# Scores of a gated linear attention: from three matmuls a chunk over zero-padded queries to eight, on two halves of TensorE's rows

## What is computed

```
for t in range(S):
    m_new = maximum(f_gate[t] + m, i_gate[t])
    f_stab = exp(f_gate[t] + m - m_new); i_stab = exp(i_gate[t] - m_new); m = m_new
    C = f_stab * C + i_stab * outer(v[t], k[t])
    n = f_stab * n + i_stab * k[t]
    y[t] = sigmoid(o_gate[t]) * (C @ q[t]) / max(|n . q[t]|, 1)
x = y as [B, S, H * D]
h = relu(x.T @ w_tok1) @ w_tok2;  u = x + h.T
out = u + relu(u @ w_ch1) @ w_ch2
```

## Time and profile before

| | us |
|---|---|
| median of three runs | 455.25 (454.03 to 457.1) |
| the profiled execution's own time | 455.49 |
| its span in the trace | 453.8 |
| TensorE (PE) busy | 439.6, 97% of the span |
| VectorE (DVE) busy | 255.6, 56% |
| ScalarE (ACT) busy | 209.1, 46% |
| GpSimd (POOL) busy | 208.3, 46% |
| granted TensorE clock | 0.995 of full |

### The profile page before, as it was taken

One profiled execution on the slowest core, in us unless ns is written; L12 is line 12 of the kernel. 1 busy time (PEld: TensorE's weight loads), 2 busy tenths in 40 slices (PEclk: granted clock), 3 DMA queues, 4 the chain that ended last, 5 costly groups with the idle time before them and its releaser, 6 DMA issues.

```text
span 453.8 us, 9518 instructions
## 1 busy us (share of the span) xinstructions
PE 439.6 (97%) x3463; PEld 407.6 (90%) x3463; DVE 255.6 (56%) x592; ACT 209.1 (46%) x517; POOL 208.3 (46%) x293
## 2 busy tenths in 40 slices
PE   8899999999999999899999999999999999999996
PEld 3588988999999989799999998899999998999996
DVE  7689865777765356776674237666665326213122
ACT  3666459666554247654552137655652213211120
POOL 7535421789886333888861204798883000000000
PEclk9899999999999999999999999999999999999999
DMA  7557990443344415434454013534310010000101
GB/s 211 195 168 217 348 263 27 119 129 111 103 131 146 127 43 166 143 92 131 124 154 143 1 44 102 150 120 142 126 61 1 1 43 2 0 1 0 46 1 43
DMA packets 36616, 47.38 MB, mean 104 GB/s; under 512 B 3356, under 2 KB 29082, under 8 KB 36570
## 3 DMA queue, kind: packets, MB, share of 16 engines
q1 hardware_dynamic: 35674, 45.76, 33.4%
q10 hardware_dynamic: 896, 1.02, 0.6%
HBM read 42.73 MB, written 4.03 MB: 103 GB/s over the span
## 4 chain that ended last, share of the span: by engine, by line
PE 85%; DVE 5%; issue 4%; ACT 4%; DMA 1%; DVEq 0%; POOL 0%; POOLq 0%; ACTq 0%
PE pC L1165 32%; PE pA L1236 7%; PE pA L1237 7%; PE pA L1238 7%; PE pS L1077 6%; PE pA L1165 5%; PE pY L1134 4%; PE pA L1240 3%; PE pA L1241 3%; PE pC L1015 2%; PE pY L1113 2%; PE pN L1089 2%; DVE gb L856 1%; PE pA L1195 1%; DMA x<-o_gate_dram 1%
## 5 line engine op out<-in xcount | busy, mean ns | idle before, releaser
L988 DVE SCALAR_TENSOR_TENSOR h_lo<-pA,h_hi 128x384 fp32r<-128x384 f32 x96 | 53.5, 557 | 147.9 <-ACT h_hi L760 147.9
L760 ACT ACTIVATE h_hi<-pA 128x384 fp32r<-128x384 f32 x96 | 46.8, 488 | 138.7 <-PE pA L1241 138.6
L1165 PE MATMUL pC<-wc_hi,h_hi 128*128 128x320 f32 x288 | 94.1, 327 | 1.1 <-DVE wc_lo L846 1.0
L1165 PE MATMUL pC<-wc_lo,h_hi 128*128 128x320 f32 x288 | 88.7, 308 | 0.0
L1165 PE MATMUL pC<-wc_hi,h_lo 128*128 128x320 f32 x288 | 88.4, 307 | 0.0
L494 POOL TENSOR_TENSOR gb<-gb,pb 128x384 f32<-128x384 f32 (+1 forms) x54 | 49.1, 909 | 63.9 <-ACT pb L628 63.4
L1236 PE MATMUL pA<-uT_hi,wc_hi 128*128 128x384 f32 x192 | 65.2, 340 | 0.3 <-DVE wc_lo L846 0.3
L1237 PE MATMUL pA<-uT_lo,wc_hi 128*128 128x384 f32 x192 | 64.7, 337 | 0.0
L1238 PE MATMUL pA<-uT_hi,wc_lo 128*128 128x384 f32 x192 | 64.3, 335 | 0.0
L1165 PEld LDWEIGHTS pC<-wc_hi,h_hi 128*128 128x128 f32 x288 | 54.0, 188 | 2.3 <-DVE h_lo L988 1.3
L1165 PEld LDWEIGHTS pC<-wc_lo,h_hi 128*128 128x128 f32 x288 | 54.2, 188 | 0.1
(11 more groups left out here) (135 smaller groups left out, 881.6 us busy)
## 6 DMA issues: line engine op xcount, KB each, us to landing
gb<-g_dram SPq DMA_DIRECT2D x18, 512.0 KB, 3.9
kv<-kvN_dram SPq DMA_DIRECT2D x24, 324.0 KB, 4.0
kd<-kT_dram SPq DMA_DIRECT2D x24, 180.0 KB
qz<-qT_dram SPq DMA_DIRECT2D x72, 60.0 KB
out_dram<-u SPq DMA_DIRECT2D x24, 160.0 KB, 1.9
qd<-qT_dram SPq DMA_DIRECT2D x20, 180.0 KB, 2.6
gq<-g_dram SPq DMA_DIRECT2D x45, 60.0 KB
wc_raw<-w_ch_dram SPq DMA_DIRECT2D x6, 384.0 KB, 6.1
```

Source lines behind the costliest of these rows:

```text
L760: nc.scalar.activation(h2[0][:, slot % 2], pA[slot % 2][:, 0:HALF], ACT.Relu).then_inc(h2_hi, 1)
L988: nc.vector.scalar_tensor_tensor(h2[1][:, slot % 2], pA[slot % 2][:, 0:HALF], 0.0, h2[0][:, slot % 2].bitcast(F32), ALU.max, ALU.subtract) ...
L1165: ins = mm(dst, a[p], b[q], start=first and n == 0, stop=last and n == 2)
```

## The change

Queries and keys now lie in one tensor `kq` with the even heads on rows 0 to 39 and the odd heads on rows 64 to 103, 128 columns for each pair of heads, keys and queries side by side. The host lays the input out that way (`kq_pairs`), and two DMAs of a chunk, 4 KB for each of 40 rows, replace the four. The memset of `qz` is gone, and SP no longer waits for it; SP loads `kq` of chunk 0 first, then the values of chunk 0, and then waits until the output gates of batch 0 have landed before it goes on with chunk 1.

All eight heads' scores of a chunk are made in the step g0 by eight matmuls of 128 columns, even and odd heads by turns. Even heads go to `pS`, odd ones to another bank: `pC[0]` in the first batch, `pN` in the others. They wait until VectorE has read all scores of the chunk before (`p_ready`), and in batches 1 to 3 also until it has read that chunk's last state.

Since `pN` holds the odd heads' scores, the states of batches 1 to 3 are written into columns of `pN` whose scores were read: group 0's in the step g1, those of groups 1 and 2 both in the step g2. VectorE reads the scores of a step in two instructions, one per bank; in g1 it first waits for the state matmul of group 0, in g2 for all three.

```diff
-        kd = sb("kd", [ROWS, R, NG, L])
-        qz = sb("qz", [ROWS, R, NG, GH, L])
+        kq = sb("kq", [128, R, 2, H // 2, L])
...
+        def scores_place(ba, head):
+            pair, odd = divmod(head, 2)
+            return (pC[0] if ba == 0 else pN) if odd else pS, pair * L
+
+        def state_place(ba, g):
+            col = L if ba > 0 and g == NG - 1 else 0
+            return pN[0:HEADS[g] * D, col:col + HEADS[g] * E1]
...
+        def states_in(ba, m):
+            if ba == 0:
+                return [m - 1] if 1 <= m <= STEPS - NG else []
+            c, g = divmod(m, NG)
+            if c >= NC - 1 or g == 0:
+                return []
+            return [m - 1] if g == 1 else [m - 1, m]
...
-                    sp.wait_ge(s_mm, NG * (n - R + 1))
+                    sp.wait_ge(s_mm, n - R + 1)
...
-                sp.dma_start(kd[:, r], kT[ba, c]).then_inc(ready, 16)
-                for j in range(GH):
-                    rows_j = slice(j * D, (j + 1) * D)
-                    sp.dma_start(qz[rows_j, r, :, j, :], queries[rows_j, :, :]).then_inc(ready, 16)
+                for odd in range(2):
+                    sp.dma_start(kq[64 * odd:64 * odd + D, r], kq_pairs[ba, c, odd]).then_inc(ready, 16)
...
+            load_scores(0, 0)
             load_values(0, 0)
-            sp.wait_ge(mem_ready, 1)
-            load_scores(0, 0)
+            for half in range(2):
+                sp.wait_ge(o_in[half], 16)
...
-            nc.vector.memset(qz[:, :, :, :, :], 0.0).then_inc(mem_ready, 1)
...
-                dve.wait_ge(s_mm, k + 1)
+                dve.wait_ge(s_mm, NC * ba + c + 1)
+                if ba > 0 and c < NC - 1 and g > 0:
+                    dve.wait_ge(n_mm, NG * (NC - 1) * ba + NG * c + (1 if g == 1 else NG))
                 dve.wait_ge(e_exp, k + 1)
...
+                for odd in range(2):
+                    heads = [h for h in range(GH * g, GH * g + n) if h % 2 == odd]
+                    tile = gb[:, c % Q, heads[0]:heads[-1] + 1:2, :]
+                    where, col = scores_place(ba, heads[0])
+                    sums = where[:, col:col + len(heads) * L].rearrange("p (h t) -> p h t", t=L)
+                    last = nc.vector.tensor_tensor(tile, sums, tile, ALU.mult)
+                last.then_inc(p_ready, 1)
...
+            def chunk_scores(ba, c):
+                n = NC * ba + c
+                r = c % R
+                pe.wait_ge(qk_in[r], 16 * QK_DMAS * (ba * (NC // R) + c // R + 1))
+                if n > 0:
+                    pe.wait_ge(p_ready, NG * n)
+                if ba > 0:
+                    pe.wait_ge(n_read, states(ba, c - 1))
+                for head in range(H):
+                    pair, odd = divmod(head, 2)
+                    rows = slice(64 * odd, 64 * odd + D)
+                    last = mm(scores_of(ba, head), kq[rows, r, 0, pair, :], kq[rows, r, 1, pair, :],
+                              start=True, stop=True)
+                last.then_inc(s_mm, 1)
...
-                if ks != 0:
+                if ba == 0 and ks != 0:
                     pe.wait_ge(n_read, ks)
+                if ba > 0:
+                    pe.wait_ge(p_ready, STEPS * ba + NG * c + (1 if g == 0 else 2))
+                    if g > 0:
+                        pe.wait_ge(n_read, NG * (NC - 1) * ba + NG * c + 1)
...
-                if m < STEPS:
-                    step_scores(ba, m)
+                if m < STEPS and m % NG == 0:
+                    chunk_scores(ba, m // NG)
```

More of the change, by code:

```diff
@@ L79, in step_in, with program @@
     return slot - BEHIND if b == 0 else slot + AHEAD
-def program(nc, qT, kT, kvN, i_gate, f_gate, o_gate, w_tok1, w_tok2, w_ch1, w_ch2, out):
+def program(nc, kq_pairs, qT, kvN, i_gate, f_gate, o_gate, w_tok1, w_tok2, w_ch1, w_ch2, out):
     ctx = ExitStack()
@@ L163, in program, with scores_of @@
         pN = bank("pN")
-        def scores_bank(ba, m):
-            return [pS, pC[0]][m % 2] if ba == 0 else pS
+        def scores_place(ba, head):
[4 more added lines that the diff above has]
+            return pN[0:HEADS[g] * D, col:col + HEADS[g] * E1]
+        def scores_of(ba, head):
+            where, col = scores_place(ba, head)
+            return where[:, col:col + L]
         def turned_bank(s):
@@ L188, in program @@
         out_done = [sem(f"out_done{i}") for i in range(2)]
-        mem_ready = sem("mem_ready")
         ident_ready = sem("ident_ready")
@@ L303, in program @@
         O_PARTS = ((0, NC - 2), (NC - 2, NC))
-        QK_DMAS = 4
+        QK_DMAS = 2
         GQ_DMAS = 3
@@ L317, in load_scores @@
                 if n >= R:
-                    sp.wait_ge(s_mm, NG * (n - R + 1))
+                    sp.wait_ge(s_mm, n - R + 1)
                 ready = qk_in[r]
-                queries = qT[ba, c]
-                sp.dma_start(kd[:, r], kT[ba, c]).then_inc(ready, 16)
-                for j in range(GH):
-                    rows_j = slice(j * D, (j + 1) * D)
-                    sp.dma_start(qz[rows_j, r, :, j, :], queries[rows_j, :, :]).then_inc(ready, 16)
+                for odd in range(2):
+                    sp.dma_start(kq[64 * odd:64 * odd + D, r], kq_pairs[ba, c, odd]).then_inc(ready, 16)
             def load_decays(ba, c):
@@ L874, in state @@
                 new, old = st[0:n * D, (c + 1) % 2, g, 0:n, :], st[0:n * D, c % 2, g, 0:n, :]
-                sums = pN[0:n * D, 0:n * E1].rearrange("p (h e) -> p h e", e=E1)
+                sums = state_place(ba, g).rearrange("p (h e) -> p h e", e=E1)
                 keep = blocks[0:n * D, 0:n, :]
@@ L928, in attention @@
                     scores(ba, m)
-                if 1 <= m <= STEPS - NG:
-                    state(ba, m - 1)
+                for done in states_in(ba, m):
+                    state(ba, done)
                 c = chunk_at(ba, m, 0) if (ba, m) != (0, NG - 1 + FIRST_LAG) else None
@@ L1086, in step_state @@
                 pe.wait_ge(v_weighed, (NC - 1) * ba + c + 1)
-                if ks != 0:
+                if ba == 0 and ks != 0:
                     pe.wait_ge(n_read, ks)
-                mm(pN[0:n * D, 0:n * E1], kv[:, r, GH * g * D:(GH * g + n) * D],
+                if ba > 0:
+                    pe.wait_ge(p_ready, STEPS * ba + NG * c + (1 if g == 0 else 2))
+                    if g > 0:
+                        pe.wait_ge(n_read, NG * (NC - 1) * ba + NG * c + 1)
+                mm(state_place(ba, g), kv[:, r, GH * g * D:(GH * g + n) * D],
                    vw[:, c % 2, GH * g:GH * g + n, :].rearrange("p h e -> p (h e)"),
@@ L1152, in attention @@
                                 spread_query_decays(k // NG + 1)
-                if 1 <= m <= STEPS - NG:
-                    step_state(ba, m - 1)
+                for done in states_in(ba, m):
+                    step_state(ba, done)
                 if lag(ba) <= m < STEPS + lag(ba):
@@ L1279, in rows, with paired @@
         return np.ascontiguousarray(padded.reshape(B, NG, ROWS, NC, L).transpose(0, 3, 2, 1, 4))
+    def paired(a):
+        return a.reshape(B, H // 2, 2, NC, L, D).transpose(0, 3, 2, 5, 1, 4)
     def by_partition(w, k):
@@ L1289 @@
     arrays = {
-        "qT": rows(q), "kT": rows(k),
+        "kq_pairs": np.ascontiguousarray(np.stack([paired(k), paired(q)], axis=4)),
+        "qT": rows(q),
         "kvN": np.ascontiguousarray(np.concatenate([tokens(k).reshape(B, S, DM), values.reshape(B, S, H * E1)], axis=2)),
```

3 lines of the change are left out of this document (removed).

## The result

The changed kernel takes 466.7 us (median of 4 runs, 465.11 to 467.19) against 454.92 us (4 runs, 454.03 to 457.1): a ratio of 1.0246, 95% interval 1.0202 to 1.029. It is slower. The forecast was 450.6 us with a range from 446.5 to 460.5; the result is outside it. The profiled execution took 467.19 us. Here and in the experiments the ratio and its interval compare with the kernel before and leave out executions more than 1.5% above the fastest of the same kernel, while medians and ranges take in all.

The account below looks back on a forecast made before the run. It took TensorE's instruction stream, except its few waits, to bound the kernel. Terms +0.1 - 3.2 - 2.0 + 0.7 - 0.6 + 0.3 = -4.7 us, from about 455.25, gave 450.6 us, range 446.5 to 460.5.

Parts of the forecast that it names:

- 1.31 us a chunk, made of 0.98 + 0.09 + 0.09 + 0.15: Scores' cost: nine time steps 0.98, entering 0.09, leaving 0.09, bare weight loads 0.15; gain 0.40 us a chunk.
- The first rival: Halves do not run side by side, loads or streaming one after another: 1.93 to 2.1 us a chunk, 458 to 462; chance 0.25.
- the last (no cost at all): Rival: mode changes cost nothing and loads stay hidden, 1.0 us a chunk, 447 us; chance 0.13.
- Chunks 2 to 5 of batches 2 and 3: Full gain of the scores in these chunks: 8 x 0.40 = -3.2 us.
- Batch 1 was to gain 1.3 us: Batch 1: five chunks gain 0.40 us each, -2.0; chunk 2, where VectorE is late, costs +0.7.
- 0.6 us to spare: At g0, VectorE's last state read was to be over by 215.3, PE to arrive at 215.9: no wait.
- the second rival: Halves run side by side, but PE waits in g2 or at g0: 454 to 457 us; chance 0.17.
- chunks 0 and 1 of batches 2 and 3: No gain, as these stretches end in PE's wait at 188.47; VectorE's extra instructions add +0.1 us.
- the slack: In g2, PE's margin behind `p_low` shrinks from 1.3 to 0.3 us; occasional waits counted as 0.3 us in all.
- The wait near 188 us: Batch 2's PE wait, which faster scores only lengthen: a sign to check, 2 us or more.
- the term "-0.6" for batch 0: Batch 0: shorter chain to the scan and earlier gates, less VectorE's 4 x 0.15 us: -0.6 us.
- The prediction's last sentence: Prediction is wrong if batch 0 loses over 1 us, since PE needs a chunk's three reads before the next.

Follow-up runs that it names:

- experiment 2: Kernel before the change, but batch 0's scores use one bank instead of two by turns: 457.88 us, ratio 1.0074.
- experiment 3: Changed kernel, but batch 0's score matmuls contract all 128 rows, same order and banks, scores come out wrong: 455.77 us, ratio 1.0025.
- experiment 6: Changed kernel with VectorE's two products of the values in batch 0 done for one head of eight: 453.67 us, ratio 0.9944.
- e5_apart: Changed kernel with all even heads' score matmuls first, then all odd ones, in all batches: 478.07 us, ratio 1.0523.
- e12_gates: Changed kernel with SP waiting for batch 0's output gates before it issues any scores or values: 470.44 us, ratio 1.0334.
- experiment 4: Changed kernel plus full-height bf16 dummy matmuls in batch 0: ten once 464.11 us, five ahead of chunks 1 to 5 458.91, two ahead of decay spreadings 458.84.
- the hybrid: Batch 0 as in the kernel before, batches 1 to 3 as in the changed kernel: 450.6 us, ratio 0.9912 against the kernel before.
- experiment 7: All even heads' score matmuls first, then all odd ones: 458.84 us in the hybrid, 478.07 us in the changed kernel.
- e14_once: Changed kernel with one block of ten full-height 512-column dummy matmuls ahead of chunk 4's scores in batch 0: 464.11 us, ratio 1.0188.
- e13_full: The run of experiment 3, the changed kernel with batch 0's scores on all 128 rows: 455.77 us, ratio 1.0025.

## Why the prediction was right and wrong

**The scores, right.** Predicted were 1.31 us a chunk, made of 0.98 + 0.09 + 0.09 + 0.15. Measured are 0.10 to enter, 1.09 for the instructions and 0.06 that the next one takes longer (0.32 us from 219.99 to 220.31, 0.26 before from 205.09 to 205.35): 1.25 us. Inside, one term was off: the halves start at the same instant, so there are eight time steps of 0.11 us and not nine, and the two steps of 0.21 us at the ends hold the bare load and the exit. By these numbers a chunk should gain 1.71 - 1.25 = 0.46 us; its period gives 12.55 - 12.15 = 0.40, the forecast, because other matmuls came out a little longer (the eight of a `hidden` 1.42 us from 222.17 on, 1.39 before from 211.36 on), for which no run gives a reason. The first rival (nothing side by side) is refuted, and so is the last (no cost at all). The first one's time was also added up wrongly: its terms give 459.4 to 462, not 458 to 462.

**Batches 1 to 3: right in sum, in part by luck.** -3.8 us were measured and -4.1 forecast. Chunks 2 to 5 of batches 2 and 3, each taken from its scores to the next chunk's, gain 3.2 us, as forecast. Batch 1 was to gain 1.3 us and gained 0.06: its chunks 0 and 1 take 0.3 and 0.6 us longer, where 0.4 less each was forecast, and chunk 2 costs 0.05 instead of 0.7. The waits are those of 0.35, 0.50 and 0.36 us above. The last is PE's wait at g0 for VectorE's state, which had "0.6 us to spare", and the one before it is the wait for `p_low` in g2. So the second rival, side by side but PE waits, is true of batch 1; over the three batches PE waits six times for `p_low`, 2.5 us, against twice and 1.6 us before. Against this stand chunks 0 and 1 of batches 2 and 3, which were to gain nothing and gained 0.5 us. In chunk 3 of batch 2 the slack was read well: it was to shrink to 0.3 us, and `p_low` (L888) runs from 226.78 for 0.58 us, PE's values start at 227.73, 0.37 us later. The wait near 188 us was to grow to 2 us or more. It did not: the same wait is again 0.78 us (until 203.41), and with three shorter ones before it the slots' waits are 1.9 us, for 1.4 before.

**Batch 0, wrong.** The failed step is the term "-0.6" for batch 0; measured +15.5. The prediction's last sentence named the condition, all three reads of a chunk before PE starts the next, but the sum gave it no price. It had no term for the granted clock either. The parts, as far as the runs separate them:

- The bank. Before, the scores of batch 0 alternated between two banks. Now a pair holds eight heads, and PE cannot run ahead of VectorE. The prediction saw VectorE "nearly full from 30 to 50 us" and charged only 4 x 0.15 us for its extra instructions, and not PE's wait. The changed kernel waits 1.13 and 1.04 us between 33 and 37 us; by experiment 2 such waits cost 2.8 us.
- The clock. It is 0.50 from 37.6 to 68.4 us, and PE works there without a gap. At most this costs 15.4 us, an estimate: 30.8 us at half clock are 15.4 us of work at full clock. By difference it is about 12: from the mark at 33.20 us to batch 0's end the changed kernel loses 14.1 us, and 2.2 of them are the two waits. In experiment 3, where it comes back after 3 us, batch 0 ends at 61.23; in experiment 6, where it holds (and VectorE has less to do), at 57.59.
- The start. The prediction counted on an earlier landing of the gates and on a shorter way to the scan at 19.53. The sigmoid came 1.7 us later and the scan at 21.77. Of this 1.4 us were left at 33.20.

The sum is 1.4 + 2.2 + 12 = 15.6 us, for 15.5 measured.

What brings the clock down and what keeps it down are two questions. Down it went behind two waits of 0.87 us or more, one close behind the other (the changed kernel, experiment 3, `e5_apart`), and it did not where they were smaller (experiment 6) or lay further apart (experiment 2). What pattern of waits it takes is open; in `e12_gates` it fell after a single long one, of 1.30 us. Down it stayed, for 31 us and more, where only half-height scores and the small matmuls of batch 0 followed, and it came back behind full-height work: the scores of experiment 3, the filler of experiment 4, the mixer's products from 65.69 us. Why the rest of batch 0's work, in part full-height too, does not bring it back is open. Batches 1 to 3 keep 1.00 with the same half-height scores, with the mixer's products between them. The Trainium skill (TensorE: Matmul & The Clock Gate, "A second HAM failure mode: psum-queue depth-cycling") describes a clock that falls when PE idles briefly and often between groups as it cycles through PSUM banks. The falls of the changed kernel and of experiment 3 agree with it; experiment 2, with as much idle time at 1.00, shows that short idling at a bank is not enough. That activity brings the clock back, as the Trainium skill has it (TensorE: Matmul & The Clock Gate, "What's actually happening"), these rows do not bear out as it stands: PE is 100% busy by its records at 0.50 for 31 us.

## What to carry to other kernels

Price a change stage by stage with the granted clock as a term of its own: a stage of small matmuls in which you take away a buffer may fall to half clock and stay there, here at about four times the price of the waits. A packing of two row halves that pays beside dense products need not pay in a stage without them, so apply it per stage, as the hybrid does. Write the halves' instructions alternately. And compare a forecast with the result batch by batch: a sum that fits can hide two terms that do not.

## What the runs showed of the hardware

- Matmuls on rows 0 to 39 and 64 to 103 stream truly together: eight pairs of 128 float32 columns in 1.09 us, starts 0.00 to 0.01 us apart (up to 0.04 in other chunks), with 0.10 us to enter. Full-height ones of the same columns took 1.86 us in experiment 3.
- A half's matmul can start ahead of the other half's that was written earlier: in the order of experiment 7 the first pN starts at 205.17, the last three pS at 205.28 to 205.50. The Trainium skill (TensorE: Matmul & The Clock Gate, "Part 3: Packing small matmuls — row/col tiling") says that matmuls start and end strictly in program order; across row halves these rows contradict it for the starts. They also contradict, for such halves, the sentence on the kernel before that each engine runs its instructions in the order written. Whether a semaphore on the last instruction written may then stand for both halves was not tried; in the changed kernel the two alternate, and their starts lie at most 0.04 us apart.
- The granted clock of 0.50 lasted for 31 us (48 us in `e12_gates`) under a PE that by its records was never idle. It ended at 68.4 us behind the mixer's 320-column products (from 65.69), in `e14_once` at 48.2 behind full-height matmuls of 512 columns (from 44.99), and in `e13_full` at 38.25 behind full-height scores (from 34.50).
